# The loads of v for batches 2 to 7 begun by POOL's queue instead of SP's, in a linear attention with two MLPs

## The chip, the cores and the metric

The kernel runs on one core of one Trainium2 chip. A core has five engines with a queue of instructions each: PE (TensorE, matmuls), DVE (VectorE), ACT (ScalarE), POOL (GpSimd) and SP (SyncE, which here only begins DMAs). Each engine takes its own instructions in the order in which they are written and waits at semaphores. The transfers that SP, ACT or POOL begin are carried out by 16 DMA engines. The metric is the device time of one execution in microseconds (us), of which the median of several runs is taken.

## What is computed

Linear attention over 8 batches of 8 heads, 576 tokens and 64 features, then two MLPs over the 8 x 576 = 4608 tokens, all in float32:

```
q_s = softmax(q, over the 64 features);  k_s = softmax(k, over the 576 tokens)
kv  = einsum('bhsd,bhse->bhde', k_s, v)           # 64 x 64 per batch and head
x   = q_s @ kv                                   # 4608 x 512 after the heads are put side by side
g   = max(x @ w_in, 0) + alpha * min(x @ w_in, 0)   # 512 -> 2048
y   = g @ w_out                                  # 2048 -> 512
h   = y @ w_in2;  solu = h * softmax(h);  z = (solu - mean) / sqrt(var + 1e-6) * g_ln   # 512 -> 1024
out = z @ w_out2                                 # 1024 -> 512
```

## The kernel before, in words

Each large matmul is made of three: the float32 operands are split in a high and a low part (`rh`/`rl`, `qTh`/`qTl`, `W1[..., 0, ...]` and `W1[..., 1, ...]`), and high x high, high x low and low x high are summed.

The program has three stages: (1) attention together with the first product x @ w_in, (2) the product with w_out in 7 partial products per pair of batches, (3) the second MLP. Only the first, up to about 424 us, has anything to do with the change.

**The first stage.** 512 of a batch's 576 tokens are its main part; the remaining 64 of all batches make up a ninth chunk. After a prologue for batch 0, a loop over c = 0 to 6 runs the 16 steps `up(c, f)` of chunk c on PE (12 matmuls each, L1602 to L1604) and puts the attention of batch b = c + 1 between them. What each engine does at which f is written out by hand, with the numbers of f in the code; nothing is scheduled by a planner. For b from 2 on (c from 1 on) PE runs `kv_product(b)` after step 9 (80 small matmuls, L1538), `qr_transpose(b)` after 11, `xr_product(b)` after 13, `x_product(b, 0)` and `(b, 1)` after 14, `x_product(b, 2)` and `(b, 3)` after 15 (L1576 to L1578). For b = 1 (c = 0) the first three stand one step later.

**What x_product waits for.** The scaled q (`QN`) is transposed in 32 x 32 blocks by DVE into `qz`; SP stores that in two halves (`store_qz`, L456) to `qz_scratch` and loads it back as 16 pieces of 64 KB (`load_qz`, L464), 8 for each half, which are counted by `qz_in[0]` and `qz_in[1]`. From each column j of four, ACT makes the high part (`q_high`, L836), then POOL the low part (`q_low`, L732; for b = 1 and j = 0, 1 DVE does, L1201), and PE's `x_product(b, j)` waits for that. Columns 0 and 1 are in the first half, 2 and 3 in the second.

**SP's queue.** In each step of the loop SP stores one tile of g (`store_g`, L434). Around it: k of batch b + 1 at f = 3 (`load_k`), the stores of qz, then q of batch b + 1 (`load_q`, three transfers), then the pieces of qz, then v of batch b + 1 (`load_v_part`, L399 and L402), one part each at f = 12 to 15 and the last after `store_g(c, 15)`. A part of v is 128 tokens' worth of 8 heads, 128 x 8 rows of 64 numbers, 256 KB; the fifth is the 64 remaining tokens, 128 KB. V has one buffer, so the first part waits for `kv_done`, the end of the kv_product before.

**POOL's queue.** For batch 0 and 1: the subtraction of the maximum from q (`q_sub`, L709), the scaling (`q_mul`, L723), mixed with the low parts of w_in (`w_low`, L727), of which `up(0, f)` waits for number f. Then `q_low(1, 2)` and `(1, 3)`, and for each batch b from 2 to 7: three `q_sub`, three `q_mul`, four `q_low`. POOL begins DMAs only in stage two, for the weights of the second MLP (L766 and L772).

The wait of PE for v in `kv_product` is on `v_in`, which each of the five parts raises by 16.

Of the kernel before, what the change touches and what calls it, by code (L numbers as in the profile page):

```python
# [26 lines left out]
def linear_attention_two_mlps(nc, q, k, v, w_in, w_out, alpha, w_in2, w_out2, g_ln, out):  # L27
    B, H, S, D = q.shape
    DM, F1 = w_in.shape
    F2 = w_in2.shape[1]  # L30
    TOK = 512
    TT = TOK // P
    REM = S - TOK
# [23 lines left out]
    with ExitStack() as ctx:  # L57
        def sem(name):
            return ctx.enter_context(nc.semaphore(name))
# [71 lines left out]
        k_in = [[sem(f"k{i}_in{n}") for n in range(3)] for i in range(2)]  # L131
        q_in = [sem(f"q_in{n}") for n in range(3)]
        v_in = sem("v_in")
        w_ld = [sem(f"w_ld{i}") for i in range(4)]
        w_hi = sem("w_hi")
        w_lo = sem("w_lo")
# [15 lines left out]
        kv_done = sem("kv_done")  # L152
# [185 lines left out]
        def rows(buf, piece):  # L338
            return flat(buf, piece).rearrange("p (r d) -> p r d", d=D)
# [32 lines left out]
        def _(sp):  # L372
# [116 lines left out]
            for c in range(B - 1):  # L489
                b = c + 1  # L490
                for f in range(NF):
                    if c == 0 and f + 4 < NF:
                        load_w(f + 4)
                    if f > 0:
                        store_g(c, f - 1)
                    if b > 1:
                        if f == 1:
                            store_kw(b)
                        if f == 2:
                            load_kb(b)  # L500
                    if f == 3 and b + 1 < B:
                        load_k(b + 1)
                    if f == (10 if c == 0 else 7):
                        store_qz(b, 0)
                    if f == (11 if c == 0 else 8):
                        store_qz(b, 1)
                        if b + 1 < B:
                            load_q(b + 1)
                    if c == 0:
                        if f == 12:  # L510
                            load_qz(b, 0, 8)
                        if f == 13:
                            load_qz(b, 8, 16)
                    elif f in (9, 10, 11, 12):
                        load_qz(b, 5 * (f - 9), min(5 * (f - 8), 16))
                    if b + 1 < B:
                        if f >= 12:
                            load_v_part(b + 1, f - 12)
                        if f == 12:
                            store_kx(b + 1)  # L520
                        if f == 13:
                            load_ky(b + 1)
                    if f == 15:
                        store_xr(b)
                    if f in WS_LOAD and ws_piece(c, WS_LOAD.index(f)) is not None:
                        load_ws(ws_piece(c, WS_LOAD.index(f)))
                    if f - 1 in WS_SPLIT and ws_piece(c, WS_SPLIT.index(f - 1)) is not None:
                        store_ws(ws_piece(c, WS_SPLIT.index(f - 1)))
                store_g(c, NF - 1)
                if b + 1 < B:  # L530
                    load_v_part(b + 1, TT)


            sp.wait_ge(xr_st, 16 * B)
            sp.wait_ge(xl_ok, 4 * B)
# [158 lines left out]
        @block.gpsimd  # L694
        def _(pool):
            nc.gpsimd.memset(ident[:, :], 0.0).then_inc(consts, 1)
            nc.gpsimd.memset(kw[:, :], 0.0).then_inc(consts, 1)
            nc.gpsimd.memset(kvh[:, :, :].bitcast(F32), 0.0).then_inc(consts, 1)
            nc.gpsimd.memset(kvl[:, :, :].bitcast(F32), 0.0).then_inc(consts, 1)
            nc.gpsimd.memset(mhalf[:, :], -0.5).then_inc(consts, 1)  # L700
            nc.gpsimd.memset(V[:, :, :, D:D + 1], 1.0).then_inc(consts, 1)
            pool.wait_ge(consts, 6)
            nc.gpsimd.affine_select(out=ident[:, :], in_=ident[:, :], compare_op=ALU.not_equal, fill=1.0,
                                    base=0, pattern=[[-1, P]], channel_multiplier=1).then_inc(consts, 1)
            pool.wait_ge(consts, 7)

            def q_sub(b, piece):
                pool.wait_ge(qmax_ok, 3 * b + piece + 1)
                nc.gpsimd.tensor_tensor(rows(Q, piece), rows(Q, piece), spread(stat(qm, piece), D),  # L709
                                        ALU.subtract).then_inc(qsub_ok, 1)  # L710

            def q_mul(b, piece):
                pool.wait_ge(qr_ok, 3 * b + piece + 1)
                if piece == 0:
                    if b > 0:
                        pool.wait_ge(qr_ps, b)
                elif b > 1:
                    pool.wait_ge(ql_first, 2)
                    pool.wait_ge(ql_ok, 4 * b - 2)
                elif b > 0:  # L720
                    pool.wait_ge(ql_ok, 4 * b)
                dst, src, scale = scaling(piece)
                nc.gpsimd.tensor_tensor(dst, src, scale, ALU.mult).then_inc(qn_ok, 1)  # L723

            def w_low(f):
                pool.wait_ge(w_hi, f + 1)
                nc.gpsimd.tensor_tensor(weight(f, 1), wst[:, f % 4, :], weight(f, 0).bitcast(F32),  # L727
                                        ALU.subtract).then_inc(w_lo, 1)

            def q_low(b, j):  # L730
                pool.wait_ge(qh_ok, 4 * b + j + 1)
                nc.gpsimd.tensor_tensor(by_token(qTl[:, j, :]), by_block(qT[:, j, :]),  # L732
                                        by_token(qTh[:, j, :].bitcast(F32)), ALU.subtract).then_inc(ql_ok, 1)

            for piece in range(3):
                q_sub(0, piece)
            for piece in range(3):
                q_mul(0, piece)
            for f in range(5):
                w_low(f)  # L740
            q_sub(1, 0)
            w_low(5)
            q_sub(1, 1)
            w_low(6)
            q_sub(1, 2)
            w_low(7)
            w_low(8)
            for piece in range(3):
                q_mul(1, piece)
                w_low(9 + piece)  # L750
            for f in range(12, NF):
                w_low(f)
            for j in range(2, KT):
                q_low(1, j)
            for b in range(2, B):
                for piece in range(3):
                    q_sub(b, piece)
                for piece in range(3):
                    q_mul(b, piece)
                for j in range(KT):  # L760
                    q_low(b, j)

            pool.wait_ge(ws_st, 16 * WS)
            for n in range(2):
                pool.wait_ge(b_used, ends(LAST_U, n))
                pool.dma_start(W2[:, n, :, :].rearrange("p a (h n) -> p (a h) n", h=2),  # L766
                               ws_dram[0:2 * KT, n, :, :].rearrange("m p n -> p m n")).then_inc(w2_in, 16)
            half = NF2 // 2
            for n in range(2):
                pool.wait_ge(b_used, ends(LAST_U, 2 + n))  # L770
                for i in range(2):
                    pool.dma_start(WO2[:, n * half:(n + 1) * half, i, :],  # L772
                                   ws_dram[2 * KT + n * half:2 * KT + (n + 1) * half, i, :, :]
                                   .rearrange("m p n -> p m n")).then_inc(wo2_in, 16)

            def x2_low(m, r):
                pool.wait_ge(x2h_ok, 4 * m + r + 1)
                nc.gpsimd.tensor_tensor(x2l[:, r % 2, :, :], x2[r], x2h[:, r % 2, :, :].bitcast(F32),  # L778
                                        ALU.subtract).then_inc(x2l_ok, 1)

            def power(m, r):
                s = r % 2
                pool.wait_ge(var_ok, 4 * m + r + 1)
                nc.gpsimd.tensor_tensor(st[:, s, 8:9], st[:, s, 7:8], mhalf[:, :], ALU.pow).then_inc(rstd_ok, 1)

            def tiles(m, last=False):
                for r in range(4):
                    if not (last and r >= 2):
                        x2_low(m + (r + 2) // 4, (r + 2) % 4)
                    power(m, r)  # L790

            x2_low(0, 0)
            x2_low(0, 1)
            tiles(0)
            with pool.Fori(1, LAST) as m:
                tiles(m)
            tiles(LAST, last=True)
# [708 lines left out]
        def _(pe):  # L1506
# [14 lines left out]

            def kv_product(b):
                pe.wait_ge(kexp_ok, 3 * b + 2)
                pe.wait_ge(v_in, 80 * (b + 1))
                if b < 2:
                    pe.wait_ge(km_ok, b + 1)
                else:
# [1 line left out]
                for j in range(KT):  # L1529
# [3 lines left out]
                    for t in range(TT + 1):  # L1533
                        rows_in = P if t < TT else REM
                        for lo in (0, D):
                            h = 2 * j + lo // D
# [94 lines left out]
            for c in range(B - 1):  # L1631
                b = c + 1
# [148 lines left out]
```

## Time and profile before

| | us |
|---|---|
| median of 3 runs | 1252.39 (1249.3 to 1252.76) |
| the profiled execution, its own time | 1252.95 |
| its span, first to last instruction | 1251.1 |
| PE busy in it | 1217.9 (97%) |
| DVE, ACT, POOL busy | 818.2, 509.1, 206.3 |
| mean granted TensorE clock | 0.993 of full speed |

Times in the rows are microseconds from the start of the span, unless marked ns. PE is TensorE's matmul side and PEld its weight load; SPq is SP's queue, whose instructions begin DMAs. Granted clock 1.00 is 2.4 GHz and 0.50 is 1.2 GHz. The DMA share is the mean busy share of the 16 DMA engines; since packets overlap it can be over 1.

### The profile page before, as it was taken

The page shows a single profiled execution, that of the slowest core. Times are in us where ns is not written, and L with a number is a line of the kernel's source. Part 1 is how long each engine was busy: PE and PEld are TensorE (multiplying, and loading weights), DVE is VectorE, ACT ScalarE, POOL GpSimd, SP SyncE. Part 2 cuts the span into 40 slices and gives each one's busy share as a digit, 9 for nine tenths or more (in the row PEclk, how much of TensorE's full clock was granted, in tenths as well). Part 3 has the DMA queues.
Part 4 walks back from the last instruction along what each step waited for, and adds up shares of the span by engine and source line. Part 5 has one row for each costly group of instructions (what it writes and reads, how often), then busy time and mean ns, then how long its engine had stood idle before and what let it go on. Part 6 is the DMA issues. An engine that isn't in the chain of part 4 may idle for free.

```text
span 1251.1 us, 16516 instructions
## 1 busy us (share of the span) xinstructions
PE 1217.9 (97%) x6129; PEld 1008.4 (81%) x6129; DVE 818.2 (65%) x1060; ACT 509.1 (41%) x720; POOL 206.3 (16%) x179
## 2 busy tenths in 40 slices
PE   7979999999999999999999999989999999999998
PEld 6768888888888787788888888877888888888887
DVE  7658586685873366878767787655655655556553
ACT  4533434434343344344344443433443344444432
POOL 4533324133241000000000000021111111111110
PEclk9989999999999999999999999999999999999999
DMA  9686887978854643362351613592544444444432
GB/s 233 213 228 215 237 269 232 271 230 232 270 172 164 228 168 132 113 215 105 118 202 59 227 68 119 164 306 84 177 144 150 148 143 139 148 144 141 144 124 76
DMA packets 208973, 217.52 MB, mean 174 GB/s; under 512 B 63480, under 2 KB 147984, under 8 KB 208784
## 3 DMA queue, kind: packets, MB, share of 16 engines
q1 hardware_dynamic: 204672, 208.30, 53.0%
q0 software_dynamic: 4192, 8.39, 2.2%
q8 instruction: 39, 0.64, 0.2%
q14 instruction: 22, 0.18, 0.0%
q10 hardware_dynamic: 48, 0.01, 0.0%
HBM read 124.84 MB, written 91.81 MB: 173 GB/s over the span
## 4 chain that ended last, share of the span: by engine, by line
PE 88%; DVE 4%; DMA 4%; SPq 2%; ACT 1%; issue 1%; POOL 0%; DVEq 0%; ACTq 0%
PE ps_y L1602 9%; PE ps_y L1603 9%; PE ps_y L1604 9%; PE ps_y L1688 5%; PE ps_y L1690 5%; PE ps_y L1692 5%; PE ps_y L1740 5%; PE ps_y L1741 5%; PE ps_y L1742 5%; PE ps_m L1716 2%; PE ps_h L1716 2%; PE ps_h L1720 2%; PE ps_m L1720 2%; PE ps_m L1715 2%; PE ps_h L1715 2%; PE ps_m L1688 2%
## 5 line engine op out<-in xcount | busy, mean ns | idle before, releaser
L1602 PE MATMUL ps_y<-X,W 128*128 128x512 f32 x576 | 228.2, 396 | 3.8 <-DVE gst L1212 2.9
L1603 PE MATMUL ps_y<-X,W 128*128 128x512 f32 x576 | 225.5, 391 | 0.0
L1604 PE MATMUL ps_y<-X,W 128*128 128x512 f32 x576 | 225.3, 391 | 0.0
L1212 DVE SCALAR_TENSOR_TENSOR gst<-gst,nslope,ps_y 128x512 f32<-128x512 f32 x144 | 104.8, 733 | 140.6 <-ACT gst L860 140.6
L860 ACT ACTIVATE gst<-ps_y 128x512 f32<-128x512 f32 x144 | 85.9, 596 | 245.0 <-PE ps_y L1604 215.1
L1602 PEld LDWEIGHTS ps_y<-X,W 128*128 128x128 f32 x576 | 108.9, 189 | 28.9 <-DVE gst L1212 3.4
L1604 PEld LDWEIGHTS ps_y<-X,W 128*128 128x128 f32 x576 | 108.9, 189 | 23.1
L1603 PEld LDWEIGHTS ps_y<-X,W 128*128 128x128 f32 x576 | 108.9, 189 | 21.9
L1688 PE MATMUL ps_y<-rh,WOc 128*128 128x512 f32 (+1 forms) x320 | 117.8, 368 | 0.4 <-DVE rl L1351 0.4
L1690 PE MATMUL ps_y<-rl,WOc 128*128 128x512 f32 (+1 forms) x320 | 117.7, 368 | 0.0
L1692 PE MATMUL ps_y<-rh,WOc 128*128 128x512 f32 (+1 forms) x320 | 117.7, 368 | 0.0
L1740 PE MATMUL ps_y<-WO,zh 128*128 128x512 f32 x288 | 112.2, 390 | 1.9 <-DVE zl L1471 1.9
L1742 PE MATMUL ps_y<-WO,zl 128*128 128x512 f32 x288 | 112.1, 389 | 0.0
L1741 PE MATMUL ps_y<-WO,zh 128*128 128x512 f32 x288 | 112.0, 389 | 0.0
L960 ACT ACTIVATE rh<-RX 128x1024 fp32r<-128x1024 f32 x54 | 57.3, 1061 | 92.7 <-PE ps_y L1692 41.8
L960 ACT ACTIVATE rh<-RY 128x1024 fp32r<-128x1024 f32 x54 | 57.3, 1062 | 89.5 <-PE ps_y L1692 58.8
L1351 DVE TENSOR_TENSOR rl<-RX,rh 128x1024 fp32r<-128x1024 f32 x54 | 66.2, 1225 | 40.3 <-ACT rh L960 40.3
L1351 DVE TENSOR_TENSOR rl<-RY,rh 128x1024 fp32r<-128x1024 f32 x54 | 66.1, 1224 | 36.1 <-ACT rh L960 36.1
L778 POOL TENSOR_TENSOR x2lb<-x2r,x2hb 128x512 fp32r<-128x512 f32 x36 | 47.1, 1308 | 258.5 <-ACT x2hb L993 258.5
L766 POOL DMA_DIRECT2D W<-ws_scratch x2 | 2.0, 990 | 416.7 <-PE ps_m L1692 412.4
L1688 PEld LDWEIGHTS ps_y<-rh,WOc 128*128 128x128 f32 x320 | 60.3, 189 | 10.6 <-issue 0.5
L1688 PE MATMUL ps_m<-rh,WOc 128*128 128x512 f32 (+1 forms) x160 | 60.5, 378 | 8.3 <-DVE rl L1351 8.3
(186 smaller groups left out, 2366.2 us busy)
## 6 DMA issues: line engine op xcount, KB each, us to landing
g_scratch<-gst SPq DMA_DIRECT2D x144, 256.0 KB, 3.0
RX<-g_scratch SPq DMA_DIRECT2D x36, 512.0 KB, 3.6
z_scratch<-zb SPq DMA_DIRECT2D x35, 512.0 KB, 2.6
zt<-z_scratch SPq DMA_DIRECT2D x140, 128.0 KB, 2.8
RY<-g_scratch SPq DMA_DIRECT2D x18, 512.0 KB, 4.5
RZ<-g_scratch SPq DMA_DIRECT2D x18, 512.0 KB, 4.5
x2r<-y_scratch SPq DMA_DIRECT2D x36, 256.0 KB, 3.1
KK<-k_dram SPq DMA_DIRECT2D x16, 512.0 KB, 6.4
```

The source lines that it names most:

```text
L960: nc.scalar.activation(t.tile(rh), t.raw(src), ACT.Copy).then_inc(bh_ok, 1)
L1212: nc.vector.scalar_tensor_tensor(gst[:, n % 3, :], gst[:, n % 3, :], nslope[:, f:f + 1], ps_y[:, f % 4, :], ALU.mult, ALU.add).then_inc(g_ ...
L1351: nc.vector.tensor_tensor(t.tile(rl), t.raw(src), t.tile(rh).bitcast(F32), ALU.subtract).then_inc(bl_ok, 1)
L1602: nc.tensor.matmul(o, W1[:, f, 0, a, :], x[:, 0, a, :], start=(a == 0), stop=False)
L1603: nc.tensor.matmul(o, W1[:, f, 0, a, :], x[:, 1, a, :], start=False, stop=False)
L1604: mm = nc.tensor.matmul(o, W1[:, f, 1, a, :], x[:, 0, a, :], start=False, stop=(a == KT - 1))
L1688: nc.tensor.matmul(o, WOc[k][:, 0, kt, cols], hi[:, s, :], start=begin, stop=False, skip_group_check=more)
L1690: nc.tensor.matmul(o, WOc[k][:, 0, kt, cols], lo[:, s, :], start=False, stop=False, skip_group_check=more)
L1692: mm = nc.tensor.matmul(o, WOc[k][:, 1, kt, cols], hi[:, s, :], start=False, stop=end, skip_group_check=more)
L1740: nc.tensor.matmul(o, zh[:, r % 2, f * P:(f + 1) * P], WO2[:, f, 0, :], start=(f == 0), stop=False)
L1741: nc.tensor.matmul(o, zh[:, r % 2, f * P:(f + 1) * P], WO2[:, f, 1, :], start=False, stop=False)
L1742: mm = nc.tensor.matmul(o, zl[:, r % 2, f * P:(f + 1) * P], WO2[:, f, 0, :], start=False, stop=(f == NF2 - 1))
```

## The change

For batches 2 to 7, SP no longer loads v. POOL begins the same five transfers for each batch: those for batch 2 behind its last `w_low` (number 15) and ahead of `q_low(1, 2)`; those for batch b + 1 (3 to 7) behind the third `q_mul(b, ...)` and ahead of `q_low(b, 0)`. The wait for `kv_done` goes with them. They raise a semaphore of their own, `v_late`, and `kv_product` waits for that from batch 2 on. The loads of v for batches 0 and 1 stay with SP.

```
+            def load_v_late(b, t):
+                if t == 0:
+                    pool.wait_ge(kv_done, b)
+                if t < TT:
+                    pool.dma_start(V[:, t, :, 0:D],
+                                 v[b, :, 0:TOK, :].rearrange("h (p t) d -> p h t d", t=TT)[:, :, t, :]).then_inc(v_late, 16)
+                else:
+                    pool.dma_start(V[0:REM, TT, :, 0:D],
+                                 v[b, :, TOK:S, :].rearrange("h p d -> p h d")).then_inc(v_late, 16)
...
             for f in range(12, NF):
                 w_low(f)
+            for t in range(TT + 1):
+                load_v_late(2, t)
             for j in range(2, KT):
                 q_low(1, j)
             for b in range(2, B):
...
                 for piece in range(3):
                     q_mul(b, piece)
+                for t in range(TT + 1):
+                    if b + 1 < B:
+                        load_v_late(b + 1, t)
                 for j in range(KT):
                     q_low(b, j)
...
                     if b + 1 < B:
-                        if f >= 12:
-                            load_v_part(b + 1, f - 12)
                         if f == 12:
                             store_kx(b + 1)
...
                 store_g(c, NF - 1)
-                if b + 1 < B:
-                    load_v_part(b + 1, TT)
...
             def kv_product(b):
                 pe.wait_ge(kexp_ok, 3 * b + 2)
-                pe.wait_ge(v_in, 80 * (b + 1))
+                if b < 2:
+                    pe.wait_ge(v_in, 80 * (b + 1))
+                else:
+                    pe.wait_ge(v_late, 80 * (b - 1))
```

**POOL's queue, before,** from the scaling of batch 1 to that of batch 2 (each row is an instruction with line, operation, output and inputs; Q, QN and qTl belong to q, W to w_in, V to v):

```order
L723 TENSOR_TENSOR QN<-Q,qr 128x4x4x64 [waits ql_ok,qr_ok]
L727 TENSOR_TENSOR W<-wst,W 128x512 [waits w_hi] x5
L732 TENSOR_TENSOR qTl<-QN,qTh 128x512 [waits qh_ok] x2
L709 TENSOR_TENSOR Q<-Q,qm 64x512 [waits qmax_ok]
L709 TENSOR_TENSOR Q<-Q,qm 128x1024 [waits qmax_ok] x2
L723 TENSOR_TENSOR QN<-Q,qr 64x512 [waits qr_ps,qr_ok]
L723 TENSOR_TENSOR QN<-Q,qr 128x4x4x64 [waits ql_ok,ql_first,qr_ok] x2
L732 TENSOR_TENSOR qTl<-QN,qTh 128x512 [waits qh_ok] x4
```

The same piece of POOL's queue, after:

```order
L719 TENSOR_TENSOR QN<-Q,qr 128x4x4x64 [waits ql_ok,qr_ok]
L733 TENSOR_TENSOR W<-wst,W 128x512 [waits w_hi] x5
L725 DMA V<-v_dram 128x8x64 [waits kv_done]
L725 DMA V<-v_dram 128x8x64 x3
L728 DMA V<-v_dram 64x8x64
L738 TENSOR_TENSOR qTl<-QN,qTh 128x512 [waits qh_ok] x2
L705 TENSOR_TENSOR Q<-Q,qm 64x512 [waits qmax_ok]
L705 TENSOR_TENSOR Q<-Q,qm 128x1024 [waits qmax_ok] x2
L719 TENSOR_TENSOR QN<-Q,qr 64x512 [waits qr_ps,qr_ok]
L719 TENSOR_TENSOR QN<-Q,qr 128x4x4x64 [waits ql_ok,ql_first,qr_ok] x2
L725 DMA V<-v_dram 128x8x64 [waits kv_done]
L725 DMA V<-v_dram 128x8x64 x3
```

Five transfers of v now stand between the low parts of w_in and `q_low(1, 2)`, and five more between the scaling of q of batch 2 and its four `q_low`; the latter repeats for batches 3 to 6.

**SP's queue, before,** in steps 11 to 13 of c = 0 (Q is the load of q of batch 2, QN are the pieces of qz of batch 1, kx belongs to the maximum of k):

```order
L374 DMA Q<-q_dram 64x8x64 [waits qn_ok]
L379 DMA Q<-q_dram 128x4x256 x2
L434 DMA g_scratch<-gst 128x512 [waits g_ok]
L464 DMA QN<-qz_scratch 32x4x128 [waits qz_st0]
L464 DMA QN<-qz_scratch 32x4x128 x7
L399 DMA V<-v_dram 128x8x64 [waits kv_done]
L438 DMA kx_scratch<-kx 128x16 [waits kx_ok]
L434 DMA g_scratch<-gst 128x512 [waits g_ok]
L464 DMA QN<-qz_scratch 32x4x128 [waits qz_st1]
L464 DMA QN<-qz_scratch 32x4x128 x7
L399 DMA V<-v_dram 128x8x64
```

The same piece after:

```order
L375 DMA Q<-q_dram 64x8x64 [waits qn_ok]
L380 DMA Q<-q_dram 128x4x256 x2
L435 DMA g_scratch<-gst 128x512 [waits g_ok]
L465 DMA QN<-qz_scratch 32x4x128 [waits qz_st0]
L465 DMA QN<-qz_scratch 32x4x128 x7
L439 DMA kx_scratch<-kx 128x16 [waits kx_ok]
L435 DMA g_scratch<-gst 128x512 [waits g_ok]
L465 DMA QN<-qz_scratch 32x4x128 [waits qz_st1]
L465 DMA QN<-qz_scratch 32x4x128 x7
L443 DMA ky<-kx_scratch 32x4x16 [waits kx_st]
```

The first part of v stood behind the first eight pieces of qz and ahead of the other eight; it is gone from there. In c = 1 to 5 all parts of v stood behind all sixteen pieces.

## Rows read from the trace of the kernel before

**Rows 1.** The page: busy time of each engine, share of the span, instructions.

```profile
PE 1217.9 (97%) x6129; PEld 1008.4 (81%) x6129; DVE 818.2 (65%) x1060; ACT 509.1 (41%) x720; POOL 206.3 (16%) x179
```

**Rows 2.** Longest wait of PE, 85 to 400: waiter, releaser: us, times, longest.

```profile
PE ps_h L1576 <- DVE qTl L1201: 5.4, 1, 5.4
```

**Rows 3.** Chain that ended last, 62 to 92: start, us, what.

```profile
78.90 5.11 DMA QN<-qz_scratch
...
85.44 0.80 PE ps_h L1576
```

**Rows 4.** Busy by stretch: PE, PEld, DVE, ACT, POOL, PEclk, DMA share, GB/s.

```profile
74.50:84.00 9.50, 5.54 (x38) 4.29 (x36) 2.98 (x6) 1.47 (x3) 0.00 (x0) 0.99 1.12 256
84.00:90.00 6.00, 4.56 (x11) 3.64 (x12) 1.77 (x3) 3.54 (x7) 1.71 (x2) 0.50 0.79 205
126.00:137.00 11.00, 11.00 (x64) 8.62 (x63) 6.02 (x12) 5.38 (x11) 2.03 (x2) 1.00 0.98 296
811.00:812.00 1.00, 1.00 (x10) 1.00 (x10) 0.90 (x2) 0.00 (x0) 0.00 (x0) 1.00 0.15 29
```

**Rows 5.** Timeline of SP's queue: start, us, what, count.

```profile
79.37 0.43 SPq L399 DMA_DIRECT2D V<-v_dram  x1
...
133.40 0.86 SPq L464 DMA_DIRECT2D QN<-qz_scratch  x1
134.30 1.02 SPq L399 DMA_DIRECT2D V<-v_dram  x1
```

**Rows 6.** Timeline of POOL: start, us, what, idle before and its releaser.

```profile
71.50 1.28 POOL L727 TENSOR_TENSOR W<-wst,W 128x512 fp32r<-128x512 f32 x1 [2.04 <-ACT W L853]
88.29 2.52 POOL L732 TENSOR_TENSOR qTl<-QN,qTh 128x512 fp32r<-128x512 f32 x2 [15.52 <-ACT qTh L836]
...
110.87 2.22 POOL L723 TENSOR_TENSOR QN<-Q,qr 128x1024 f32<-128x1024 f32 x1 [0.40 <-DVE qr L1184]
134.97 2.54 POOL L732 TENSOR_TENSOR qTl<-QN,qTh 128x512 fp32r<-128x512 f32 x2 [21.88 <-ACT qTh L836]
137.80 2.67 POOL L732 TENSOR_TENSOR qTl<-QN,qTh 128x512 fp32r<-128x512 f32 x2 [0.29 <-ACT qTh L836]
...
344.89 2.54 POOL L732 TENSOR_TENSOR qTl<-QN,qTh 128x512 fp32r<-128x512 f32 x2 [1.57 <-ACT qTh L836]
```

**Rows 7.** Timeline of PE: kv_product(1), then x_product in later batches.

```profile
63.03 3.58 PE L1538 MATMUL ps_m<-V,KK 128*64 128x65 f32 x80
...
139.44 0.39 PE L1576 MATMUL ps_h<-qTh,kvh 128*128 128x512 f32 x1
...
143.53 0.39 PE L1576 MATMUL ps_m<-qTh,kvh 128*128 128x512 f32 x1
...
349.34 0.39 PE L1576 MATMUL ps_m<-qTh,kvh 128*128 128x512 f32 x1
```

**Rows 8.** Chain that ended last, 0 to 450: kv_product(2).

```profile
120.79 3.52 PE ps_m L1538 x80
```

**Rows 9.** DMA from 144 to 145, while parts of v move: packets, queue's share.

```profile
DMA packets 1029, 0.29 MB, mean 291 GB/s; under 512 B 1011, under 2 KB 1011, under 8 KB 1029
...
q1 hardware_dynamic: 1029, 0.29, 122.5%
```

**Rows 10.** POOL's DMAs: two groups (busy us, mean ns); the first in the timeline.

```profile
L772 POOL DMA_DIRECT2D WO<-ws_scratch x4 | 3.0, 747 | 9.1 <-PE ps_y L1692 4.9 <-PE ps_h L1692 4.3
L766 POOL DMA_DIRECT2D W<-ws_scratch x2 | 2.0, 990 | 416.7 <-PE ps_m L1692 412.4 <-PE ps_y L1692 4.4
...
809.64 1.10 POOL L766 DMA_DIRECT2D W<-ws_scratch  x1 [412.35 <-PE ps_m L1692]
```

**Rows 11.** Landing of SP's RX loads (512 KB): 700 to 809, then 820 to 838.

```profile
DMA to landing us min/median/max: 3.4/3.6/4.6
...
DMA to landing us min/median/max: 6.8/8.3/9.8
```

**Rows 12.** SP's transfers of v, 60 to 400: landing.

```profile
DMA to landing us min/median/max: 2.9/3.8/6.1
```

More of the change, by code:

```diff
@@ L133, in linear_attention_two_mlps @@
         v_in = sem("v_in")
+        v_late = sem("v_late")
         w_ld = [sem(f"w_ld{i}") for i in range(4)]
```

## The prediction

> **What bounds the kernel now.** The busy times come first: PE works 97% of the span and every other engine has time to spare [rows 1]. So only what makes PE wait, or run at its lower clock, can cost or give time. PE's waits, longest first, come next. In the stretch from 85 to 400, in which the loop over the batches runs, there is one wait worth the name, 5.4 us of `x_product(1, 0)` for the low part of its q [rows 2]; from 126 to 137 PE is busy for all 11.00 us of 11.00 [rows 4]. The chain of waits then tells what lies behind the 5.4 us: a transfer of 5.11 us, the eighth piece of the first half of qz, which SP had issued by 78.90, then a step each on ACT and DVE, then PE at 85.44 [rows 3]. PE's clock falls with that wait: from 84 to 90 the granted clock is 0.50, the lower level of 1.2 GHz [rows 4].
>
> The change touches this in two ways: parts of v leave SP's queue, and they come onto POOL's, earlier than before. PE does not wait for v: `kv_product(2)` starts at 120.79 [rows 8]; the parts of batch 3 begin at 134.30 at SP [rows 5] and are wanted one batch later. An earlier v is worth nothing in itself. What counts is what v's issues do to POOL, and what its packets do to the qz pieces.
>
> **What leaves SP.** 30 issues, 5 for each of batches 2 to 7. In c = 1 to 5 SP's v stood behind the last piece of qz (133.40, then v at 134.30) [rows 5], so that no piece comes sooner, and PE waited for nothing there. In c = 0 the first part of v stood at 79.37 behind the eight pieces of the first half and ahead of the second [rows 5]: the critical first half is issued no sooner. The second half gains an issue of 0.43 us, which PE does not wait for. Direct gain: 0.
>
> **What POOL gets: the issues.** The nearest row is POOL's own transfer of `W`, 128 x 8 rows like a part of v: 990 ns each; the half as large ones take 747 ns [rows 10]. Five parts are 4 x 0.99 + 0.75 = 4.7 us. Three places:
> - Batch 2: POOL ends its last `w_low` at 71.50 + 1.28 = 72.8 [rows 6]. The wait for `kv_done` is over: `kv_product(1)` ended at 63.03 + 3.58 = 66.6 [rows 7]. POOL issues from 72.8 to 77.5; its next work starts at 88.29 [rows 6]. Hidden, with 10.8 us left.
> - Batches 3 to 7: `q_mul` of batch 2 ends at 110.87 + 2.22 = 113.1 [rows 6]; then POOL waits for `kv_product(2)`, until 120.79 + 3.52 = 124.3 [rows 8]. Behind this added wait stand the four `q_low` of the batch and, through them, `x_product`. POOL is ready again at 124.3 + 4.7 = 129.0, and `q_low(2, 0)` can start at 134.97 at the earliest, for ACT [rows 6]. Hidden, with 6.0 us left. PE wants that part at 139.44 [rows 7], so `q_low` (2.54 / 2 = 1.27 us each) may start at 138.17: an issue may take (138.17 - 124.3) / 5 = 2.8 us before PE waits.
> - Batch 0 and 1: nothing changes.
>
> **What POOL gets: the packets.** Here is the real cost. All queues share the DMA engines. In SP's queue v stood behind the qz pieces; from another queue it runs beside them. While parts of v moved in the old kernel, 1029 packets went by in 1 us at a DMA share of 122.5% [rows 9]: I take that as full. v of a batch has 4 x 1024 + 512 = 4608 packets (one for each row of 256 bytes), so it takes 4608 / 1029 = 4.5 us of all engines.
>
> First place, c = 0. POOL issues from 72.8. Its transfer of W issued at 809.64 had few packets (29 GB/s) from 811 to 812 [rows 4, 10], so v moves from about 74.5. From 74.5 to 84.0 the share was 1.12 [rows 4]; against 1.225, 9.5 x 0.105 / 1.225 = 0.8 us is spare. The one part of v that SP used to begin at 79.37 is no longer in that stretch, 1024 / 1029 = 1.0 us. The first half of qz lands later by 4.5 - 0.8 - 1.0 = **2.7 us**, and PE waits 8.1 us in place of 5.4. From below: with the part of v gone and v moving in time that packets leave free, -1.0. From above: SP's loads of RX landed after 8.3 us (middle) beside POOL's big transfers, 3.6 without them, so +4.7 [rows 11]; the worst of them was 9.8, +6.2. I take 2.7, since it is worked out from the very stretch and the RX loads met 2 KB packets. The clock costs nothing more, as I assume: it falls at about 84 anyhow, and the stretch at 0.50 [rows 4] moves with PE's new start.
>
> The Trainium skill, "DMA: Bandwidth & Descriptors", section "Queues, rings and completion order", speaks against this change too: each DMA engine takes turns, packet by packet, between the queues that have work. By that rule no more packets of v can go ahead than SP's queue has packets of its own, so that the delay is at most that of as many packets of v, not of a whole batch of v; the RX loads agree in sign (8.3 against 3.6 us [rows 11]). Where SP has fewer than 4608 packets ahead of the last piece this lowers my 2.7 somewhat.
>
> Five later places, c = 1 to 5. v moves from about 126. From 126 to 137 the share was 0.98 [rows 4], so 11 x 0.245 / 1.225 = 2.2 us is spare and the second half of qz, the last piece of which SP issues at 133.40, lands 4.5 - 2.2 = 2.3 us later. `q_low` of column 2 started at 137.80 [rows 6] and takes 1.27, ending at 139.1; PE wants it at 143.53 [rows 7]: 4.4 us of room. The least room is in c = 5: 344.89 + 1.27 = 346.2 [rows 6] against 349.34 [rows 7], 3.2 us. The 2.3 us are hidden. If the cover failed, PE would lose all that lies over 3.2 to 4.4 us, five times.
>
> **Sum.** 0 for SP, 0 for POOL's issues, 2.7 for the first half of qz of batch 1, 0 for the five later places. PE never makes up for a wait once lost there, so all 2.7 us reach the end. The profiled execution took 1252.95, 0.56 above the median of the runs, 1252.39. 1252.95 + 2.7 = 1255.65 for it, 1255.1 for the median. A difference under 0.3%, 3.8 us, is about what a measurement of this kernel can't tell from none.
>
> **Rivals.**
> 1. **v's packets find room.** The moved bytes in 74.5 to 84 are only 256 GB/s [rows 4], less than the 291 GB/s of a stretch with rows of 256 bytes [rows 9] and 296 GB/s from 126 to 137. Against it: the share there is 1.12, near full. Then the first half of qz lands between 1.0 us sooner and 0.5 later: 1251.4 to 1252.9. No change.
> 2. **The five later places break through,** the one that ends slower. The second half of qz is delayed by the full cost or more, 4.5 to 6.2 us (the worst RX load [rows 11]), and PE loses what is over 3.2 to 4.4. It decides from a delay of 3.2 us. At 4.5 it is some 0.5 us on average, five times; at 6.2 it is 2.2, five times: 2.5 to 11 us, with 2.7 to 4.7 for the first place: 1258 to 1268. For it: two RX loads did land that late. Against it: by 133.40 most of v is through if it began at 126.
> 3. **POOL's issues are long.** They decide from 2.8 us for one. If POOL holds each until it has landed, 3.8 us as SP's did [rows 12], POOL is free at 124.3 + 19 = 143.3, PE 5.1 us late in five batches: 26 us, with the first place 1281. Against it: POOL's transfers of W lasted 0.99 us on POOL while 2 MB of each had yet to move [rows 10].
> 4. **Faster.** The first half of qz lands so much earlier that PE starts before its clock falls at 84, that is 1.4 us sooner or more, and the time from 84 to 90 at 1.2 GHz [rows 4] goes too: half of some 5 us, 2.5, and 1.5 or more of the wait: 1248.4. Only if one part of v was what held the pieces up, and 4608 packets beside them do not.
> 5. **The change doesn't do what it says:** the five parts per batch are begun by POOL before the pieces of qz in either queue, as the order shows; I leave this out.
>
> **How the numbers follow.** Forecast, 0 to 4.7 us more with 2.7 in the middle: 0.58. Rival 1: 0.15. Rival 2: 0.17. Rival 3: 0.05. Rival 4: 0.05. Of the forecast's 0.58, 0.40 lies under 3.8 us and 0.18 above. So faster 0.05, same 0.40 + 0.15 = 0.55, slower 0.18 + 0.17 + 0.05 = 0.40. The range: from 1251.0 (rival 1's gain, with the runs' own spread) to 1263 (half of rival 2), which leaves out rivals 3 and 4 and part of 2, together under 0.2.
>
> **What the profile of the changed kernel would show.** The wait of PE for `qTl` in `x_product(1, 0)`: 8.1 us by the forecast, 4.4 to 5.9 by rival 1. POOL's issues of v in two groups, 72.8 to 77.5 and from 124.3, each about 1 us; over 2.8 is rival 3. No wait of PE at `x_product(b, 2)` for b = 2 to 6; five such waits are rival 2. The transfer of the last piece of the first half of qz in the chain: 7 to 8 us in place of 5.11. If PE's other waits change, or the wait at 80 is shorter, I was wrong on how v's packets share the engines.

## The result

| | before | after |
|---|---|---|
| median, us | 1251.02 (4 runs, 1249.3 to 1252.76) | 1266.99 (4 runs, 1265.62 to 1271.39) |
| ratio | | 1.0134, 95% interval 1.0103 to 1.0165 |
| profiled execution, us | 1252.95 | 1265.62 |
| span | 1251.1 | 1263.8 |
| PE busy | 1217.9 | 1222.0 |

The change makes the kernel 1.3% slower: 16 us between the medians. The two profiled executions are only 12.7 us apart, since that of before is the slowest of its four runs and that of after the fastest; the readings below explain those 12.7.

The longest waits of PE from 85 to 400 in the kernel after (waiter, releaser: us in total, times, longest us). One stood there before [rows 2], three stand there now:

```profile
PE ps_h L1590 <- DVE qTl L1212: 9.3, 1, 9.3
PE ps_h L1590 <- POOL qTl L738: 3.0, 8, 0.6
PE ps_m L1590 <- POOL qTl L738: 2.8, 7, 1.1
```

The first is `x_product(1, 0)`, 5.4 us before. The other two are the `x_product` of later batches, in both halves: ps_h takes columns 0 and 1, ps_m columns 2 and 3. The chain that ended last shows what was behind them, in the stretch from 62 to 200 (start, us, what); it answers [rows 3] and [rows 8]:

```profile
78.33 8.58 DMA QN<-qz_scratch
86.93 0.64 ACT qTh L847
87.59 0.70 DVE qTl L1212
88.34 0.79 PE ps_h L1590
...
122.92 3.52 PE ps_m L1552 x80
...
136.18 8.49 DMA QN<-qz_scratch
144.69 0.64 ACT qTh L847
145.40 2.55 POOL qTl L738 x2
147.99 0.50 PE ps_m L1590
...
176.15 3.52 PE ps_m L1552 x80
```

The last piece of the first half of qz of batch 1 lands 8.6 us after SP's issue instead of 5.1, and the last piece of batch 2 lands 8.5 us after its issue. In the kernel before, no piece of qz stands in the chain after batch 1. The distance of one `kv_product` to the next says what a batch takes: 53.2 us here. From 120.79 to 378.06 in the kernel before, five batches took 51.45 us each; from 122.92 to 390.88 now they take 53.59:

```profile
326.61 3.52 PE ps_m L1538 x80
378.06 3.52 PE ps_m L1538 x80
```

(kernel before, the last two of its chain) and

```profile
390.88 3.52 PE ps_m L1552 x80
```

(kernel after). Five times 2.14 is 10.7 us; up to `kv_product(2)` the two are 122.92 - 120.79 = 2.1 apart. Together 12.8; the spans differ by 12.7. The 2.1 hide a little of the first place, because this execution of the kernel after was 1.0 us ahead at `kv_product(1)`, before the change could act (62.02 against 63.03):

```profile
62.02 3.58 PE L1552 MATMUL ps_m<-V,KK 128*64 128x65 f32 x80
```

From one `kv_product` to the other the first place costs 3.1 us in this pair of traces.

The recorded waits of the later batches add up to only 5.8 us, and the spacing is the better measure. At such a wait more is lost than is recorded. The first low part of batch 2 is a case (kernel after; start, us, what, idle before):

```profile
141.34 0.39 PE L1618 MATMUL ps_y<-X,W 128*128 128x512 f32 x1
141.99 0.50 PE L1590 MATMUL ps_h<-qTh,kvh 128*128 128x512 f32 x1 [0.26 <-POOL qTl L738]
142.33 0.39 PE L1591 MATMUL ps_h<-qTl,kvh 128*128 128x512 f32 x1
```

From the first to the third of these starts 0.99 us pass, and 0.45 us in the kernel before (139.22 to 139.67): 0.54 us are lost where 0.26 are recorded. Fifteen waits with 0.28 us more each make an estimate of 10.0 us, near the 10.7.

POOL's timeline after, with the new issues (start, us, what, idle before), answers [rows 6]:

```profile
71.56 3.76 POOL L725 DMA_DIRECT2D V<-v_dram  x4
75.29 0.72 POOL L728 DMA_DIRECT2D V<-v_dram  x1
89.85 2.51 POOL L738 TENSOR_TENSOR qTl<-QN,qTh 128x512 fp32r<-128x512 f32 x2 [13.84 <-ACT qTh L847]
...
126.74 3.57 POOL L725 DMA_DIRECT2D V<-v_dram  x4 [11.53 <-PE ps_m L1552]
130.30 0.70 POOL L728 DMA_DIRECT2D V<-v_dram  x1
140.65 2.52 POOL L738 TENSOR_TENSOR qTl<-QN,qTh 128x512 fp32r<-128x512 f32 x2 [9.65 <-ACT qTh L847]
```

The issues cost POOL 4.5 us at the first place and 4.3 at the later ones, less than the 4.7 expected, and POOL sat idle for 9.65 us behind them until ACT had its part. It was the pieces that were late.

### The profile page after: what moved, and what is told of

It reads as the page before. It is cut to its first block, busy times and chain, and to the rows that moved or that the text cites. A ratio compares the mean times of both kernels' runs of the same rounds, so it can differ in the third digit from the quotient of the medians.

```text
span 1263.8 us, 16516 instructions
## 1 busy us (share of the span) xinstructions
PE 1222.0 (97%) x6129; PEld 1006.1 (80%) x6129; DVE 815.8 (65%) x1060; ACT 507.8 (40%) x720; POOL 231.9 (18%) x209
## 3 DMA queue, kind: packets, MB, share of 16 engines
q1 hardware_dynamic: 176544, 201.22, 50.3%
## 4 chain that ended last, share of the span: by engine, by line
PE 77%; DMA 8%; DVE 7%; SPq 5%; issue 1%; ACT 1%; POOL 1%; DVEq 0%; ACTq 0%
PE ps_y L1616 6%; PE ps_y L1617 6%; PE ps_y L1618 6%; PE ps_y L1702 5%; PE ps_y L1706 5%; PE ps_y L1704 5%; PE ps_y L1754 5%; PE ps_y L1756 5%; PE ps_y L1755 5%; DMA QN<-qz_scratch 4%; PE ps_h L1734 2%; PE ps_m L1729 2%; PE ps_m L1734 2%; PE ps_h L1729 2%; PE ps_m L1730 2%; PE ps_h L1730 2%
## 5 line engine op out<-in xcount | busy, mean ns | idle before, releaser
L1702 PEld LDWEIGHTS ps_y<-rh,WOc 128*128 128x128 f32 x320 | 60.3, 189 | 11.7 <-issue 1.8
L1706 PEld LDWEIGHTS ps_y<-rh,WOc 128*128 128x128 f32 x320 | 60.3, 189 | 10.1
```

Source lines behind the costliest of these rows:

```text
L1702: nc.tensor.matmul(o, WOc[k][:, 0, kt, cols], hi[:, s, :], start=begin, stop=False, skip_group_check=more)
L1706: mm = nc.tensor.matmul(o, WOc[k][:, 1, kt, cols], hi[:, s, :], start=False, stop=end, skip_group_check=more)
```

## The experiments

Theory: v's transfers are harmless in themselves; what they cost is what they put on the DMA engines beside or ahead of the pieces of qz, and that is lost only as far as it exceeds the room behind the pieces. Rivals: POOL's queue as such; the size of its packets; POOL's issues or its new wait; one place dragging the others. The times are medians; ratios are against runs of the kernel before on the same chip (its medians 1250.5 to 1251.2).

| run | v begun by, when | median | ratio, 95% interval |
|---|---|---|---|
| after | POOL, early | 1266.99 | 1.0134 (1.0103 to 1.0165) |
| pool_late | POOL, behind the low parts of q | 1251.53 | 1.0005 (0.9996 to 1.0014) |
| sp_early | SP, early | 1269.2 | 1.0156 (1.0142 to 1.017) |
| act_early | ACT, early | 1295.83 | 1.0373 (1.0358 to 1.0387) |
| pool_first_early | POOL, batch 2 early | 1256.17 | 1.0049 (1.0035 to 1.0062) |
| act_first_early | ACT, batch 2 early; POOL late for the others | 1255.12 | 1.0038 (1.0025 to 1.0051) |
| pool_rest_early | POOL, batches 3 to 7 early | 1261.53 | 1.0082 (1.0063 to 1.0101) |
| pool_two_early | POOL, two of five parts of batches 3 to 7 early | 1250.92 | 1.0003 (0.9994 to 1.0013) |
| q_behind | SP as before, q of batch 2 behind the pieces | 1247.93 | 0.998 (0.9971 to 0.9989) |
| q_behind_pool | pool_late and q_behind together | 1248.47 | 0.9975 (0.9964 to 0.9986) |
| q_behind_together | the same, 16 pieces at once | 1250.69 | 0.9997 (0.9988 to 1.0006) |

**pool_late: the same queue, later.**

```
             for j in range(2, KT):
                 q_low(1, j)
+            for t in range(TT + 1):
+                load_v_late(2, t)
...
                 for j in range(KT):
                     q_low(b, j)
+                for t in range(TT + 1):
+                    if b + 1 < B:
+                        load_v_late(b + 1, t)
```

(and taken away from where the change put them)

> The changed kernel with POOL's transfers of v moved behind the low parts of q: for batch 2 behind q_low(1, 3), for batch b + 1 behind q_low(b, 3). Same queue, same issues, only later. Theory (v's packets from POOL's queue stand between the pieces of qz and delay them): nothing moves beside the pieces any more, the wait of PE for qTl in x_product(1, 0) is back at 5.4 us, no wait at x_product(b, 2), time within 3 us of the kernel before (about 1251 to 1252). Rival (what POOL's queue costs is its issues, or POOL's descriptors as such, wherever they stand): still 10 us or more slower than before.

Measured: 1251.53, not to be told from before. The wait in `x_product(1, 0)` is 3.9 us in its trace. Its batches are 51.45 us apart again:

```profile
117.36 3.52 PE ps_m L1552 x80
168.81 3.52 PE ps_m L1552 x80
```

All 30 issues are still POOL's. So POOL's queue, its issues and the fewer entries in SP's queue together are worth nothing measurable; the moment is.

**sp_early: one queue, as early.** In step 12 of c = 0 and in step 10 later (the calls of `load_v_part` are taken away):

```
+                    if b + 1 < B and f == (12 if c == 0 else 10):
+                        load_v(b + 1)
                     if c == 0:
                         if f == 12:
                             load_qz(b, 0, 8)
```

> The kernel before with v begun as early by SP itself: for batch 2 ahead of the sixteen pieces of qz in step 12 of c = 0, for batch b + 1 in step 10, ahead of pieces 5 to 15. One queue only, all of v's packets ahead of the pieces. Theory of my prediction (v costs its 4.5 us of engine time, less what is spare, plus five issues of 0.45 us at SP): the first half of qz of batch 1 lands some 5 to 6 us later, and the later ones 3 to 5 us, of which 3 to 4 are hidden: 1256 to 1262. If only a second queue beside SP's is harmful: 1251 to 1254.

Measured: 1269.2, worse than POOL and outside my 1256 to 1262. The direction says that no second queue is needed for the loss. The size has a reason of its own, in SP's timeline in c = 0 (start, us, what, count):

```profile
73.44 6.42 SPq L399 DMA_DIRECT2D V<-v_dram  x4
79.91 2.39 SPq L402 DMA_DIRECT2D V<-v_dram  x1
82.34 3.94 SPq L464 DMA_DIRECT2D QN<-qz_scratch  x8
```

Five issues took SP 8.9 us where I had put 5 x 0.45. The pieces were issued 7.4 us later than before (82.34 against 74.96) and then landed within 2.6 us. What makes an issue long isn't shown: the single part of v that the kernel before issued at 79.37 took 0.43 us, in a stretch (78 to 84) with a DMA share of 1.23.

**act_early: another queue, packets of 256 bytes.** `load_v_late` on ACT, with the same semaphore:

```
                     negative(c, f)
+                    if b + 1 < B and f == (12 if c == 0 else 9):
+                        for t in range(TT + 1):
+                            load_v_late(b + 1, t)
```

> The changed kernel with the same transfers of v at about the same times, but begun by ACT's queue: for batch 2 behind the negative part of step 12 of c = 0 (about 73 us), for batch b + 1 behind that of step 9, when kv_product(b) has ended. It too is a queue beside SP's, but its packets should be the 256-byte rows that SP's v has (a batch of v brings 4608 packets; in the changed kernel POOL's queue brings 368, so 16 rows to most packets). Theory of the large packets (an engine takes turns by packet, so a piece's packet of 512 bytes waits for one of 4096 bytes): with 256-byte packets the pieces are delayed far less, time 1251 to 1256. Rival (any queue beside SP's with this load at this time costs the same, since the bytes or the engine time count): 1262 to 1268 as with POOL, and packets landing 8 us after issue.

Measured: 1295.83, far above both. The run doesn't tell what it was made for, because ACT itself is in the way. ACT's timeline (start, us, what, idle before):

```profile
125.57 7.17 ACTq L805 DMA_DIRECT2D V<-v_dram  x4
132.77 2.91 ACTq L808 DMA_DIRECT2D V<-v_dram  x1
135.79 0.60 ACT L866 ACTIVATE gst<-ps_y 128x512 f32<-128x512 f32 x1 [13.14 <-issue]
```

Ten microseconds of issues stopped ACT's other work, and PE waited for what hangs on it (line of its waits up to 450):

```profile
PE ps_m L1563 <- DVE kvf L1164: 32.8, 6, 7.5
```

**pool_first_early and pool_rest_early: the two places apart.** The first keeps the transfers for batch 2 where the change has them and moves the others behind `q_low(b, 3)`; the second does the opposite.

> The changed kernel with only the transfers for batch 2 where the change puts them; those for batches 3 to 7 stand behind the low parts of q. Splits the loss by place. By the chain of the two traces the first place costs 3 to 4 us (the wait in x_product(1, 0) 9.3 us in place of 5.4) and the five later ones 9 in sum: expected 1254 to 1256. If the later ones are harmless by themselves and only follow from the first (through a shifted order of SP): 1264 to 1268.

> The changed kernel with the transfers for batch 2 moved behind q_low(1, 3) and those for batches 3 to 7 left where the change puts them. The other half of the split: the first place alone cost 1256.2 against 1250.5, 5.7 us; the whole change 16. If the two are independent: 10 us slower than before, 1260 to 1262, kv_product 53.2 us apart in place of 51.45. If the later places only lose because the first has shifted something: 1251 to 1253.

Measured: 5.7 us and 11 us over before. Their sum, 16.7, agrees with the 16.0 of the whole change: the places add up. In pool_first_early the later batches are 51.45 us apart (124.13, 175.59 and so on) and the wait in `x_product(1, 0)` is 9.9 us. pool_rest_early's runs spread more than the others (1257.12 to 1264.57), so its share is known to some 2 us. Its trace has one batch that lost nothing, from 226.51 to 277.97, 51.46 us:

```profile
226.51 3.52 PE ps_m L1552 x80
277.97 3.52 PE ps_m L1552 x80
```

It is the batch in which three of the five parts of v were issued only 6.7 us after the first two, by a pause of POOL (last section). In the kernel after the same batch is the shortest of the five, 52.7 us, and has no wait on ps_h.

**act_first_early: the packets' size once more,** with ACT's v for batch 2 alone, on a semaphore of its own.

```
+                    if c == 0 and f == 12:
+                        for t in range(TT + 1):
+                            load_v_late(2, t)
```

> v of batch 2 alone begun by ACT at about 71 us (4608 packets of 256 bytes in a queue of their own), v of batches 3 to 7 by POOL behind q_low. Beside pool_first_early (368 packets, 4096 bytes most of them, 1256.2) it tells what the packets' size is worth, with ACT's own delay in it, which the run with all of v on ACT showed to be 8 us at this place. If the size decides: pieces of the first half land 10.5 to 12.5 us after DVE's last transpose of q, time 1251 to 1253. If the amount decides: 14.5 to 16.5 us after, 1254 to 1258.

Measured: 1255.12 against 1256.17 with POOL's large packets; the intervals overlap. The first half of qz was there 14.9 us after DVE's last transpose (ACT's next work at 85.59, DVE done at 70.67), 16.6 us in pool_first_early (87.32 and 70.71), 12.1 before. So the same amount in small packets still delays the half by 2.8 us, against 4.5 in large ones. Whether the other 1.7 us are the packets' size isn't shown: these are single executions, ACT issued v over 8.4 us where POOL took 4.5, and a difference between the two times isn't shown either. ACT was held up for 8 us besides, and PE waited 3.2 us for it ahead of `x_product`.

**pool_two_early: a part of the load.**

```
+                for t in range(2):
+                    if b + 1 < B:
+                        load_v_late(b + 1, t)
                 for j in range(KT):
                     q_low(b, j)
+                for t in range(2, TT + 1):
+                    if b + 1 < B:
+                        load_v_late(b + 1, t)
```

> The transfers for batch 2 late, and of those for batches 3 to 7 only the first two parts early, the other three behind q_low. Theory of a delay that grows with what is put beside the pieces and is free up to the room of 3.2 to 4.4 us: 2048 of 4608 packets delay the last piece by 0.44 of the 5.8 us measured, 2.6 us, which is hidden: within 2 us of before, 1250 to 1252. Rival (POOL's queue as such upsets the pieces, or the wait of POOL for kv_done does, in proportion): 0.44 of the loss or all of it, 1255 to 1261.

Measured: 1250.92, no loss. The last piece of batch 2 lands 4.8 us after its issue; before it was 3.3 at most, in the changed kernel 8.5. POOL has its added wait for `kv_done` here too (11.53 us), and its two issues, and neither costs anything. The loss is what exceeds the room, not a share of the load.

**q_behind: the same reasoning turned on the kernel before.**

```
-                        if b + 1 < B:
+                        if b + 1 < B and c > 0:
                             load_q(b + 1)
...
                             load_qz(b, 8, 16)
+                            load_q(b + 1)
```

> The kernel before with one edit that follows from the same reasoning: in c = 0 the load of q of batch 2 (1.15 MB, three transfers, wanted at 98 us) no longer stands ahead of the sixteen pieces of qz but behind them. If what stands ahead of the pieces in the DMA engines sets PE's wait, the wait of 3.9 to 5.4 us in x_product(1, 0) falls to under 2 us and PE's clock stays at 2.4 GHz there: 4 to 7 us faster than before, 1243 to 1247. If the pieces are slow by themselves (rows of 512 bytes from scratch): no more than 1.5 us faster.

Measured: 1247.93, 0.2% faster, less than the 4 to 7 us expected. The two longest waits for qTl in batch 1 (PE's waits, 20 to 440):

```profile
PE ps_h L1577 <- DVE qTl L1202: 1.5, 1, 1.5
PE ps_m L1577 <- POOL qTl L733: 1.3, 1, 1.3
```

The mechanism came true: the pieces land 1.9 to 3.1 us after issue in place of 4.4 to 5.6, the wait of the first half falls to 1.5 us and the clock stays at 1.00. But 1.3 us come back at the second half, which nothing had shown as close. And the profiled execution of before, with its 5.4 us of wait, took 1252.95, against a median of 1250.5; in pool_late and pool_two_early, where nothing of v is early at this place, PE waited 3.9 and 4.0 us.

**q_behind_pool and q_behind_together.** The first is q_behind on pool_late. The second issues all sixteen pieces in step 12 (`load_qz(b, 0, 16)`).

> pool_late with the load of q of batch 2 behind the sixteen pieces of qz in c = 0: nothing but stores of g stands beside the pieces in either queue. SP's first part of v, which stood between the halves, is gone too. If all that stands ahead of or between the pieces counts: a little faster than q_behind (1247.9), by up to the 0.5 us of that issue: 1246.5 to 1248. If POOL's later v has a price of its own: 1248 to 1250.

> As q_behind_pool, with all sixteen pieces issued in step 12 of c = 0, ahead of the stores of kx and of the next tile of g, so that the second half is issued from 75.3 instead of 77.8. q_behind's waits in batch 1 were 1.5 us for the first half and 1.3 for the second; the second should go: 1245 to 1247, 0.3% to 0.4% under before. If the store of g then comes too late for its buffer instead: no gain over q_behind_pool.

Measured: 1248.47 and 1250.69. The first can't be told from q_behind. The second gives the gain back by the rival named for it: the store of g behind the pieces comes too late for its buffer. ACT's timeline:

```profile
88.29 0.60 ACT L870 ACTIVATE gst<-ps_y 128x512 f32<-128x512 f32 x1 [3.77 <-DMA g_scratch<-gst]
```

That wait stands ahead of the last two columns of x on ACT, and PE then waits 2.5 us at the first matmul of the next chunk. Its clock falls behind that wait (0.72 on average from 90 to 96).

## Why the prediction was wrong

**Right.** PE did not wait for v. SP gained nothing. POOL's issues were hidden: 0.89 and 0.69 us in the middle against the 0.99 and 0.75 I took, far from the 2.8 us at which they would have counted (rival 3). What costs is the pieces of qz, and both places that I named are the two places of loss.

**Wrong: the forecast that the later places are covered.** I put 1255.1 and 1251 to 1263; it is 1267.0 and rival 2, which I gave 0.17, at the upper end of its 1258 to 1268. The step that failed is the delay of the pieces there, 4.5 us for v less 2.2 us spare, 2.3 us, under a room of 3.2 to 4.4. Measured: landing 8.5 in place of 3.3, and the issue 0.65 us later than PE's shift explains, together 5.8 us. Both terms were off. So was my ground against rival 2, that most of v is through by 133.40. In the kernel after v's parts are issued from 126.74 on, and the last, issued at 130.30, lands 9.3 us later, at 139.6 (transfers issued from 126 to 140: KB each, median us to landing):

```profile
V<-v_dram POOLq DMA_DIRECT2D x4, 256.0 KB, 7.6
V<-v_dram POOLq DMA_DIRECT2D x1, 128.0 KB, 9.3
```

*The spare time.* I had taken the DMA share of 122.5% [rows 9] as full and so 0.98 as 80% [rows 4]. The share in the same stretch of the kernel after, and in the stretch that lies as far behind `kv_product(2)` as 126 to 137 did before (PE, PEld, DVE, ACT, POOL, PEclk, DMA share, GB/s):

```profile
126.00:137.00 11.00, 11.00 (x58) 8.77 (x55) 7.21 (x13) 3.31 (x7) 4.26 (x5) 1.00 1.05 262
128.10:139.10 11.00, 11.00 (x64) 8.62 (x63) 5.74 (x11) 3.31 (x7) 2.90 (x4) 1.00 1.10 250
```

With 1.18 MB more to move, the share rose from 0.98 to 1.05 and 1.10, but the engines moved less, 262 and 250 GB/s against 296. pool_two_early has two parts of v there, pool_late none, at the same distance from `kv_product(2)` (the first line is pool_late):

```profile
122.50:133.50 11.00, 11.00 (x64) 8.59 (x63) 5.95 (x12) 5.31 (x11) 1.96 (x2) 1.00 0.91 293
122.50:133.50 11.00, 11.00 (x63) 8.60 (x63) 5.92 (x12) 5.05 (x10) 2.46 (x3) 1.00 1.11 303
```

The share rose by 0.20 and the rate by 10 GB/s, 0.11 MB in 11 us, where 0.52 MB of v had come in. SP's queue moved 2.79 MB in place of 3.21, and its packets took 89.9% of the engines' time in place of 90.8%: beside v the same share stands for fewer bytes. So the distance of the share from 1.225 told nothing of how much more could be moved: of bytes, almost nothing more was. That the mark came from a stretch in which almost only rows of 256 bytes move may be the reason; no run tests it.

*v's own time.* By queue, 126 to 140 (packets, MB, share of the engines' time), kernel after:

```profile
q1 hardware_dynamic: 2750, 2.30, 67.0%
q0 software_dynamic: 368, 1.18, 39.1%
```

and kernel before:

```profile
q1 hardware_dynamic: 6025, 3.96, 97.6%
```

39.1% of 14 us is 5.5 us, not 4.5. And while v was there, SP's queue moved 2.30 MB in place of 3.96. 5.5 us with nothing spare is close to what the last piece was late by (5.8); that is an agreement of sums, not a test of how the engines share. Over the room of 3.2 to 4.4 the 5.8 are 1.4 to 2.6 us a batch; the batches grew by 2.14.

**Missed: the first half in later batches.** I gave room only to the second half and to POOL's issues. Column 0 had 3.2 us (138.17 less 134.97); in the kernel after its low part starts at 140.65, which is 5.7 later, 2.1 of them PE's own shift, and PE waits there as well (8 of the 15 waits are on ps_h). So the rooms of 3.2 to 4.4 us were not the only ones.

**The first place.** Forecast +2.7. The time from the end of DVE's last transpose (71.88 before, 70.89 after) to ACT's next work went from 12.1 to 16.0 us, so +3.9 in this pair; pool_first_early has 5.7 us between medians. The terms were v's 4.5 us, 0.8 spare and 1.0 for part 0 of v. The first two are those that failed in the later places. Whether the 1.0 was right is open: with part 0 gone and no v early, the last piece of the first half lands after 3.7 us in pool_late and pool_two_early but after 5.2 in pool_rest_early, and after 5.1 before. The bound of +4.7 from the RX loads [rows 11] would have been the better value.

That 3.9 and 5.7 differ lies in good part with the executions. From `kv_product(1)` to `kv_product(2)` it takes 57.7 us in the trace of before, but 55.3, 55.7 and 56.9 in pool_late, pool_two_early and pool_rest_early, where v of batch 2 is late, and 60.8 and 62.2 in the kernel after and in pool_first_early, where it is early. Between these groups lie 4 to 7 us.

**The clock.** I had it cost nothing more, as the stretch at the lower level was to move with PE's new start. It didn't move along. In the kernel after the clock fell earlier (PEclk in the columns as above):

```profile
81.00:82.00 1.00, 0.00 (x0) 0.00 (x0) 0.00 (x0) 0.00 (x0) 0.00 (x0) 0.79 1.07 238
82.00:91.00 9.00, 2.66 (x6) 2.15 (x7) 2.04 (x3) 3.61 (x7) 1.15 (x1) 0.50 0.88 250
91.00:92.00 1.00, 1.00 (x4) 0.78 (x3) 0.77 (x2) 0.64 (x2) 1.00 (x2) 0.59 0.17 40
```

It was at 1.2 GHz until about 91.8, of which PE, starting at 88.34, worked for 3.5 us. Before it was there from about 83.8 to 90.6, and PE, starting at 85.44, worked for 5.2 us of it ([rows 4]; 0.69 on average from 90 to 91). From PE's start to `kv_product(2)` it took 34.6 us in place of 35.4: in this pair 0.8 us of the longer wait came back. That is not so in each execution. In pool_first_early the lower level lasts until 94, PE works for 5.3 us of it, and the same way takes 35.4 us:

```profile
84.00:94.00 10.00, 5.27 (x12) 4.14 (x13) 3.33 (x5) 4.14 (x8) 2.51 (x2) 0.50 0.72 181
```

**The rule of taking turns by packet** ("DMA: Bandwidth & Descriptors" of the Trainium skill, section "Queues, rings and completion order") I had read as a limit to v's share, with packets of one row. POOL's packets are not of one row (below), so equal turns would give v more, not less. No run here decides how the turns go: with packets of 256 bytes on ACT's queue the first half was late by 2.8 us in place of 4.5, with ACT's slower issues in it.

## What to carry to other kernels

Before a transfer is moved, ask what it will pass or stand beside, and how late that may come: here 1.18 MB beside sixteen small loads cost 11 us in five places from POOL's queue, ahead of them in SP's queue it cost time too, and behind them nothing. Don't count DMA time as spare from a share measured with other transfers: here the share still rose, from 0.91 to 1.11, while the bytes moved hardly did. Unless a stretch with the same mix moves more bytes, price the delay by v's whole time. And list the room of every consumer of the delayed transfers, not only of the one with the latest load.

The best versions, q_behind and q_behind_pool, are 0.2% to 0.25% faster than the kernel before, which comes from moving a load that nobody needed yet behind the ones that PE was waiting for.

## What the runs showed of the hardware that was not expected

- By the traces' count, POOL's queue puts 16 rows of 256 bytes into a packet, SP's and ACT's put one. The 27,648 rows of v for six batches plus 480 (16 for each of 30 transfers) were 28,128 packets of SP's queue (204,672 before, 176,544 after) and are 1728 + 480 = 2208 of POOL's (4192 before, 6400 after); 27,648 / 1728 = 16. A row of the large weights, 2 KB, was a packet of its own there (4096 rows and 16 for each of six transfers, 96, are the 4192).
- POOL's issues last 0.88 to 1.10 us for 1024 rows in all traces, early or late. For the same transfer SP's and ACT's took 0.37 to 0.38 us at best, and up to 4.1 us (sp_early) and 4.5 us (act_early) when several of v stood one behind another. On ACT that stops its arithmetic.
- In the kernel after POOL stood for 6.46 us between two of its issues of v with nothing to wait for in the trace. It lies between the second and the third part of v of batch 5, which are its 17th and 18th issues of v:

```profile
233.59 1.81 POOL L725 DMA_DIRECT2D V<-v_dram  x2 [11.53 <-PE ps_m L1552]
241.86 1.77 POOL L725 DMA_DIRECT2D V<-v_dram  x2 [6.46 <-issue]
```

  The pause comes again behind the 17th issue, with 15,872 rows issued, in pool_rest_early (6.70 us), pool_late (4.62), pool_first_early (4.45), q_behind_pool (4.59) and q_behind_together (4.42). In act_first_early, where POOL's first issues are those for batch 3, it has moved to batch 6, and is behind the 17th issue again:

```profile
295.99 1.81 POOL L726 DMA_DIRECT2D V<-v_dram  x2
303.73 1.76 POOL L726 DMA_DIRECT2D V<-v_dram  x2 [5.93 <-issue]
```

  So it goes with what POOL has issued, not with the place in the program. In pool_two_early POOL does other work and waits between these two issues, and no pause shows. What causes it is open. It did no harm: in the kernel after `q_low` of that batch starts 10.7 us behind the first issue (244.33), in the other four 13.9 to 14.3 us.
